# Expert weights made into f16 parts while attention runs, for three f16 products in place of one in f32

## The reference

```python
# attention with a state per head; B, H, S, D = 4, 8, 768, 48
k_n = k / (np.linalg.norm(k, axis=-1, keepdims=True) + 1e-06)
for t in range(S):
    y[:, :, t] = einsum('bhd,bhde->bhe', q[:, :, t], state)
    v_old = einsum('bhde,bhd->bhe', state, kt)
    state = state + bt * einsum('bhd,bhe->bhde', kt, vt - v_old)
# experts; x = y as (3072, 384); E = 8, F = 1024; expert_idx = argmax of normed logits
for e in range(E):
    h = np.maximum(x[mask] @ w1[e], 0.0)
    out[mask] = gate_w[mask, None] * (h @ w2[e])
# MLP, 384 -> 2048 -> 384
h = np.maximum(x @ w_in, 0.0)
return h * h @ w_out
```

## Time and profile before

| | us |
|---|---|
| three runs, median (lowest, highest) | 1134.9 (1131.6, 1136.0) |
| the profiled execution | 1133.4 |
| its span, first to last instruction | 1131.6 |
| attention, to the last of TensorE's work in it | 0 to 418.6 |
| experts, from `up`(0) | 421.4 to 735 |
| MLP | 735 to 1131.6 |
| TensorE, VectorE, ScalarE, POOL busy in the span | 1064.5, 674.0, 586.5, 322.5 |
| DMA share in attention, 100 to 400 us | 0.20 to 0.35 |

### The profile page before, as it was taken

How to read it: one execution, slowest core, us unless ns; L and a number is a source line. 1 busy time by engine, 2 the same in 40 slices (tenths; PEclk the granted TensorE clock), 3 DMA queues, 4 the chain that set the end, 5 groups by cost and what they waited for, 6 DMA issues and landing times. The chain is left out here.

```text
span 1131.6 us, 25343 instructions
## 1 busy us (share of the span) xinstructions
PE 1064.5 (94%) x10332; PEld 828.0 (73%) x10332; DVE 674.0 (60%) x1381; ACT 586.5 (52%) x1229; POOL 322.5 (28%) x292
## 2 busy tenths in 40 slices
PE   3799999999999879999999999879999999999998
PEld 1577888888887769999999999835555555555554
DVE  4788888888888626675557656634343434344333
ACT  2577677776777644555556656523332433333332
POOL 4466767777666632100002100041010100000000
PEclk9899999999999979999999999979999999999999
DMA  6122123332331055998656416131010100000000
GB/s 116 22 42 47 32 43 72 79 87 61 76 85 45 16 172 194 372 393 296 246 198 202 168 46 248 39 87 30 29 30 1 44 15 29 1 28 1 28 1 28
DMA packets 119091, 106.03 MB, mean 94 GB/s; under 512 B 78072, under 2 KB 108480, under 8 KB 118976
## 3 DMA queue, kind: packets, MB, share of 16 engines
q1 hardware_dynamic: 108976, 80.56, 23.9%
q0 software_dynamic: 5536, 17.50, 4.7%
q10 hardware_dynamic: 4464, 6.35, 1.5%
HBM read 129.90 MB, written 21.68 MB: 134 GB/s over the span
## 5 line engine op out<-in xcount | busy, mean ns | idle before, releaser
L1758 PE MATMUL mlp_ps<-xg_t,win 128*128 128x512 f16 x864 | 202.5, 382 | 1.0 <-DVE xg_t L1857 1.0
L1769 PE MATMUL mlp_ps<-wout,sq_hl 128*128 128x384 f16 x1128 | 197.0, 326 | 0.0
L1364 PE MATMUL expert_ps<-xs_t,w_sb 128*128 128x128 f32 x1488 | 173.7, 277 | 1.3 <-issue 0.6
L1364 PEld LDWEIGHTS expert_ps<-xs_t,w_sb 128*128 128x128 f32 x1488 | 172.7, 194 | 2.3 <-issue 1.4
L1769 PEld LDWEIGHTS mlp_ps<-wout,sq_hl 128*128 128x128 f16 x1128 | 110.4, 98 | 81.9
L1758 PEld LDWEIGHTS mlp_ps<-xg_t,win 128*128 128x128 f16 x864 | 85.0, 99 | 94.2 <-issue 2.8
L1864 DVE TENSOR_TENSOR sq<-relu 128x512 f32<-128x512 f32 x96 | 66.5, 693 | 138.6 <-ACT relu L1807 132.0
L1478 DVE TENSOR_TENSOR w_hl<-w_sb,w_hl 128x1536 fp32r<-128x1536 f32 x62 | 108.6, 1753 | 54.4 <-ACT w_hl L1413 54.4
L1375 PE MATMUL expert_ps<-w_hl,ht_hl 128*128 128x384 f32 x744 | 137.5, 339 | 0.6 <-issue 0.6
L839 DVE TENSOR_TENSOR p_cur<-newt,cst 128x256 f16<-128x256 f32 x288 | 109.0, 419 | 45.9 <-PE newt L453 42.5
L1807 ACT ACTIVATE relu<-mlp_ps 128x512 f32<-128x512 f32 x96 | 57.3, 597 | 147.4 <-PE mlp_ps L1758 147.4
(11 more groups left out here) (226 smaller groups left out, 1642.9 us busy)
## 6 DMA issues: line engine op xcount, KB each, us to landing
w_sb<-in_moe_w SPq DMA_DIRECT2D x62, 1536.0 KB
sorted_y<-ys ACTq DMA_DIRECT2D x31, 200.0 KB
xs<-sorted_x SPq DMA_DIRECT2D x31, 192.0 KB
k_raw<-in_k SPq DMA_DIRECT2D x24, 192.0 KB, 3.0
q_pad<-in_q SPq DMA_DIRECT2D x24, 192.0 KB, 3.9
v_raw<-in_v SPq DMA_DIRECT2D x24, 192.0 KB, 4.0
sorted_x<-zeros SPq DMA_DIRECT2D x11, 384.0 KB, 4.1
out<-o_sb SPq DMA_DIRECT2D x5, 768.0 KB, 3.5
```

Of the source, the lines that this page charges most:

```text
L1364: mm = pe.matmul(ps[:, 1 + half, c * P:(c + 1) * P], w1_sb[j % 2][:, kd, f], xs_t[:, kd], start=(kd == 0), stop=(kd == KD - 1))
L1758: mm = pe.matmul(ps[:, 4 + f % 2, :], win[:, a, kd, f * P:(f + 1) * P], xg_t[:, par, b, kd], start=(kd == 0 and a + b == 0), stop=(kd == K ...
L1769: mm = pe.matmul(ps[:, t, 0:DM], sq_hl[:, f % RING, a, t * P:(t + 1) * P], wout[:, b, f], start=(f == 0 and a + b == 0), stop=(f == K2 - 1 ...
```

## The change

w1 of every expert (24 chunks of 128 x 1024) is loaded twice more during attention, one chunk in an iteration. The first load is squared by ScalarE (`square_weight`); TensorE sums the squares of an expert over the partitions (`weight_sum`); VectorE makes a factor from the sum (`weight_factor`). The second load is scaled by VectorE (`scale_weight`), cast to its high f16 part by ScalarE (`high_weight`), and POOL subtracts to get the low part (`low_weight`). SP stores both parts to `w1_hl` in DRAM and, at the end, the factors. As buffers they use what the experts stage later loads w2 and w1 of its first tile into. x gets a factor of its own per row: VectorE makes it (`x_factor`), ScalarE applies it (`scale_x` in place of the second copy of y), and it travels as a 385th column.

In the experts, w1 comes in as the two f16 parts and its factor. `up` does (high, high), (low, high), (high, low): 72 f16 products in place of 24 in f32. VectorE makes x's low part (`low_x`), multiplies the two factors (`scale_back`), and `keep_y` has one more one-column operation. VectorE's order of a tile changes: `low_w2(j, 1)`, which stood at the end of tile j-1, now stands between `low_h(j, 0)` and `low_h(j, 1)`. Several semaphores are merged.

```diff
@@ attention, SP @@
+        def load_squared(i):
+            ...
+            sp.dma_start(w_sq[:, i % W_RING], w1[e, kd * P:(kd + 1) * P, :]).then_inc(s_w_sq_in, 16)
+        def load_split(i):
+            ...
+            wait(sp, s_w_lo, i - KD + 1)
+            sp.dma_start(raw_chunk(i), w1[e, kd * P:(kd + 1) * P, :]).then_inc(s_w_in, 16)
+        def store_split(i):
+            ...
+            sp.wait_ge(s_w_lo, i + 1)
+            wait(sp, s_w_out, 16 * i)
+            sp.dma_start(w1_hl[e][:, 0:sh.W1]..., rt.w1_sb[0][:, 0:sh.W1]...).then_inc(s_w_out, 16)
         for n in range(2, NP):
             load(n)
+            if n >= 3:
+                load_squared(n + 1)
+                load_split(n - 3)
+                store_split(n - 6)
+        for n in range(NP, NP + 6):
+            load_split(n - 3)
+            store_split(n - 6)
+        sp.wait_ge(s_w_factor, 3 * E)
+        sp.wait_ge(s_w_out, 16 * W_ALL)
+        sp.dma_start(w1_hl[:, :, sh.W1:sh.W1 + 2]..., w_factor[:, :, :]).then_inc(s_w_out, 16)
         rt.load_x(sp, sorted_x, 0)
         e = rt.expert(sp, 0)
-        rt.load_w1(sp, w1, e, 0)
         rt.load_w2(sp, w2, e, 0)
+        sp.wait_ge(s_w_out, 16 * (W_ALL + 1))
+        rt.load_w1(sp, w1_hl, e, 0)
@@ attention, POOL @@
+            pool.wait_ge(s_w_hi, i + 1)
+            pool.tensor_tensor(w_hl[:, 1, i % KD], raw_chunk(i), w_hl[:, 0, i % KD], ALU.subtract).then_inc(s_w_lo, 1)
             difference(n - 1)
+            low_weight(n - 2)
             low_part(n - 1)
@@ attention, ScalarE @@
-            act.copy(y_tile[:, :], y_ps[:, 0:DM])
-            wait(act, rt.s_scatter[n % RING], 16 * (n // RING))
-            act.copy(x_all[:, n % RING, :], y_ps[:, 0:DM]).then_inc(s_y, 1)
+            act.copy(y_tile[:, :], y_ps[:, 0:DM]).then_inc(s_y, 1)
             keep_logits(n - 2)
+            keep_weight_sum(n)
+            square_y(n - 2)
             store_turned(n + 1, 3)
+            high_weight(n - 1)
             newton_t(n, 4)
             newton_tt(n, 5)
-            square_y(n - 2)
+            scale_x(n - 2)
             store_turned(n + 2, 1)
+            square_weight(n)
@@ attention, VectorE @@
             lead(n - 2, 0)
+            scale_weight(n - 1)
             newton_p(n, 4)
             new_state(n - 1)
+            x_factor(n - 2)
+            weight_factor(n)
             sum_k(n + 3)
@@ experts @@
-                    for kd in range(KD):
-                        mm = pe.matmul(ps[:, 1 + half, c * P:(c + 1) * P], w1_sb[j % 2][:, kd, f], xs_t[:, kd],
-                                       start=(kd == 0), stop=(kd == KD - 1))
+                    for a, b in ((0, 0), (1, 0), (0, 1)):
+                        for kd in range(KD):
+                            mm = pe.matmul(ps[:, 1 + half, c * P:(c + 1) * P], w1_hl_sb[j % 2][:, a, kd, f], xs_hl[:, b, kd],
+                                           start=(a + b + kd == 0), stop=(b == 1 and kd == KD - 1))
+        def low_x(j):
+            ...
+            dve.tensor_copy(x_scale[:, j % 2:j % 2 + 1], xs[j % 2][:, DM:DM + 1]).then_inc(s_x_scale, 1)
+            dve.wait_ge(s_xt_hi, j + 1)
+            dve.tensor_tensor(xs_hl[:, 1], ps[:, 0, 0:DM]..., xs_hl[:, 0], ALU.subtract).then_inc(s_xt, 1)
         for j in range(NS):
             low_h(j, 0)
+            if j > 0:
+                low_w2(j, 1)
+            scale_back(j)
             low_h(j, 1)
+            if j + 1 < NS:
+                low_x(j + 1)
             ...
             if j + 1 < NS:
                 low_w2(j + 1, 0)
             keep_y(j)
-            if j + 1 < NS:
-                low_w2(j + 1, 1)
```

226 lines of the change are left out of this document (195 added, 31 removed).

## The result

The changed kernel takes 1149.7 us (median of 4 runs, 1148.7 to 1150.4), the kernel before 1135.3 (4 runs): a ratio of 1.0131, 95% interval 1.0105 to 1.0156. It is slower by 1.3%, where -0.5% was forecast; 1149.7 lies at the edge of the range. The profiled execution has a span of 1146.9 us against 1131.6, so 15.3 us are to be found in it. The two traces are held against each other at four points of TensorE's order: the start of the first `up`, the first and the last of the 31 `down`, and the end.

The account below looks back on a forecast made before the run. TensorE's own instructions were taken to bound the expert stage, VectorE and TensorE in turn attention. Terms: -40.5 (`up`) + 22 (attention) + 6.5 (gap) + 5 (VectorE) + 2 (transfers) = -5 us, giving 1129 us, range 1110 to 1150.

Parts of the forecast that it names:

- What VectorE gets in the expert stage: Expert tiles: VectorE's added work exceeds the shorter tile only with table steps or dense splits; +5 us, bounds 0 and 10.
- high_h(0) to U + 2.8, low_h(0) to U + 3.5: Expert tile: forecast end times in us, counted from U, the start of `up`; 0.3 us of cover left before `down`.
- Rival 5: Expert stage: VectorE sets every tile at 9.1 us, as low x waits for ScalarE's copy; 17 us, 1146; chance 0.05.
- transfers: Run of new experts: seven tiles in a row fall behind by 0.3 to 0.8 us each; +2 us, bounds 0 and 7.
- Rival 3: New-expert run's transfers cost 7 us and the read back of w1 4 more: 1138; chance 0.12.
- `up`: Expert tile: 72 f16 products at 56 ns take 4.01 us, 1.35 less a tile; 30 tiles give 40.5 us.
- rival 4: Expert `up`: weight loads and products do not overlap, 85 ns each; `up` 6.12 us, the whole 1192; chance 0.04.
- attention +22: Attention: 22 tiles longer by 0.36 (x's factor), 0.14 (x1's delay) and 0.3 (norm chain), plus 4.4 for weight factors.
- The norm chain's stall: Attention: VectorE's norm operations on two SBUF tensors meet POOL's low_weight; +0.3 us a tile, bounds 0 and 0.9.
- rival 2: Attention: VectorE's chunk scaling waits for POOL's port or runs slowly, 0.8 us a tile, 17.6 us: 1147; chance 0.22.
- faster is 0.39: Stated chance of a faster kernel: the forecast's faster half (0.22) with the rival of better hidden attention work (0.15).
- the gap: Between attention and experts: w1's last part is made, stored and read back; first `up` +6.5 us, bounds +1 and +11.

Follow-up runs that it names:

- the runs of the later store: Changed kernel with tile j's y stored after the first half of the next tile's high_h: 1142.0 us; the same without new weights' bytes: 1126.9 us.

## Why the prediction was wrong

**The step that failed** is "What VectorE gets in the expert stage": +5 us, bounds 0 and 10. It measured 12.0. The work was counted well (9.05 us forecast for a tile with a dense split, 8.64 found), and it would have cost next to nothing. The order "high_h(0) to U + 2.8, low_h(0) to U + 3.5" left out an instruction that issues no work: ScalarE's store of y, ahead of high_h, which waits for VectorE's last operation of the tile. In the tile above low_h(0) ends not at U + 3.5 but at U + 5.1 (U = 646.48, end at 651.54). The store was harmless while y ended at 645.90 and the products 0.5 us later; with VectorE full it closes a circle, VectorE to ScalarE to VectorE, of 1.04 us. Six tiles with dense splits lose 1.1 us each, three with table steps 3.8 together, the others 1.5 in all. Rival 5 had VectorE setting tiles, but for another reason (and its 1146 adds 17 us to a forecast that has 5 of them already).

**The second**, and the larger in size: transfers, +2 us, bounds 0 and 7. They measured 13.4. Of the 20.3 us between forecast and profile these are 11.4, VectorE's term 7.0. Rival 3 had the mechanism; the term was mis-sized. Seven new sets of 3.54 MB were held against 8.53 us. Left out were the dense pieces (0.5 MB in each of tiles 9 to 14), which the same rows 11 stretch does not show because it lies ahead of them, and the fills of sorted_x; with a piece the tile moves 4.1 MB, 10.2 us at 402 GB/s. A late set can cost clock too: in tiles 6 and 13 of the changed kernel, where TensorE waited 1.90 and 2.36 us, the clock then fell for 3.4 us and `up` took 5.81 instead of 4.20.

**Right**: `up` (4.01 forecast, 4.03 measured; 30 tiles 40.5 against 38.7, which has VectorE's tile 4 in it); no tile of rival 4. The first `up`, forecast at no gain, took 1.3 us less. The Trainium skill's rate for such a stream ("TensorE: Matmul & The Clock Gate", Back-to-back issue gap, about 81 ns at 128 columns) does not hold here: 56 ns.

**Right in part by luck**: attention +22, against 20.2 in this profile and 25 in the mean of ten. The forecast had 0.8 us a tile and 0.2 for the factors, all on the path, and no term for the clock. Undisturbed tiles grew by 0.80 in all, and about 4 of the 20.2 us are one tile whose clock fell. Of the parts, x's factor costs 0.25 us in an undisturbed tile, not 0.36 (7.8 in all, with the start of attention and one tile whose clock fell). The norm chain's stall was 0.61 us instead of 0.3, and it hit the chain's first operation, which has one input, not those on two SBUF tensors that the prediction named; on the path it was worth 0.26. Scaling was 0.74 to 1.48 against 0.6 to 1.1. The argument against rival 2, that GpSimd's scatter needs no tensor, did not hold: beside the scatter's issue the scaling took 1.31 us and more. Yet it costs the tile 0.12 and not 0.8, so rival 2's time (1147) is near the result for another reason, with attention as forecast already in it. Among the chances, "faster is 0.39" adds 0.22 and 0.15, which is 0.37.

**Within its bounds**: the gap, +6.5, measured 8.9; the factor store went out at 435.9 and w1 at 439.45, but w1 then took 11.0 us instead of the 6.3 reckoned with; the second tile's sets, requested from 443.4 on, share the engines with it.

The sum by what was measured (the experts' parts by the runs of the later store, the rest in the two profiles): -38.7 + 12.0 + 13.4 + 20.2 + 8.9 - 1.3 (the first `up`) + 0.8 (the rest) = +15.3.

## What to carry to other kernels

When an engine gets fuller, follow not its busy time but the loop that its results run through: an in-order queue that issues a store ahead of the next tile's first work couples the two engines, and this costs nothing until the feeding engine has no slack. When tiles get shorter, count every byte that lands in the stretch, side loads and fills too, against the shorter tile; at a DMA share near 1 before, a faster TensorE gets only a part of its gain. And weigh the preparation: here 38.7 us of faster products paid for 29 us of attention and gap and 25 of lost cover.
